# The normaliser multiplied into the gate on GpSimd: one multiplication moved off VectorE in a fused mLSTM and two-MLP kernel

## The reference, cut to what matters

```python
for t in range(S):
    m_new = np.maximum(f_gate[:, :, t] + m, i_gate[:, :, t])
    f_stab = np.exp(f_gate[:, :, t] + m - m_new)
    i_stab = np.exp(i_gate[:, :, t] - m_new)
    m = m_new
    C = f_stab[:, :, None, None] * C + i_stab[:, :, None, None] * np.einsum('bhd,bhe->bhde', vt, kt)
    n = f_stab[:, :, None] * n + i_stab[:, :, None] * kt
    h_tilde = np.einsum('bhde,bhe->bhd', C, qt)
    nq = np.einsum('bhd,bhd->bh', n, qt)[:, :, None]
    denom = np.maximum(np.abs(nq), 1.0)
    o = 1.0 / (1.0 + np.exp(-o_gate[:, :, t]))
    y[:, :, t] = o * h_tilde / denom
...
x = moe(x):  h = x @ w_in; g = np.maximum(0.01 * h, h); g @ w_out
x = moe2(x): h = x @ w_in; g = h * np.cos(h);           g @ w_out
```

## Time and profile before

| | |
|---|---|
| median of 3 runs | 845.6 us (844.89 to 846.51) |
| the profiled execution | 844.61 us, of it 842.9 in the span |
| TensorE busy | 832.1 us (99%) |
| VectorE, ScalarE, GpSimd busy | 626.5, 477.6, 309.2 us |

### The profile page before, as it was taken

One profiled execution on the slowest core, in us unless ns is written; L12 is line 12 of the kernel. 1 busy time (PEld: TensorE's weight loads), 2 busy tenths in 40 slices (PEclk: granted clock), 3 DMA queues, 4 the chain that ended last, 5 costly groups with the idle time before them and its releaser, 6 DMA issues.

```text
span 842.9 us, 15370 instructions
## 1 busy us (share of the span) xinstructions
PE 832.1 (99%) x5610; PEld 818.8 (97%) x5610; DVE 626.5 (74%) x1186; ACT 477.6 (57%) x1048; POOL 309.2 (37%) x340
## 2 busy tenths in 40 slices
PE   8999999999999999999999999999999999999997
PEld 7899999999999999999999999999999999999997
DVE  7598776676776666766654488888888888888886
ACT  6354433443433434334436687777777777777776
POOL 6764632222222332322005653333333333333332
PEclk9899999999999999999999999999999999999999
DMA  8764622434424224235013330301020202020000
GB/s 262 245 195 133 190 91 93 137 116 139 150 95 137 92 91 137 91 98 199 1 51 119 116 110 1 118 1 71 1 72 1 71 1 71 1 71 2 14 12 24
DMA packets 38450, 76.23 MB, mean 90 GB/s; under 512 B 3434, under 2 KB 27498, under 8 KB 38378
## 3 DMA queue, kind: packets, MB, share of 16 engines
q1 hardware_dynamic: 38330, 75.23, 27.4%
q10 hardware_dynamic: 48, 0.05, 0.0%
HBM read 63.28 MB, written 11.99 MB: 89 GB/s over the span
## 4 chain that ended last, share of the span: by engine, by line
PE 94%; DVE 1%; DMA 1%; ACT 1%; issue 1%; POOL 1%; SPq 0%; POOLq 0%; ACTq 0%; DVEq 0%
PE h L584 32%; PE acc L596 13%; PE acc L598 13%; PE acc L597 13%; PE s L584 10%; PE x L561 5%; PE s L507 3%; PE x L568 2%; PE x L549 2%; PE s L535 1%; DMA e_dram<-r_f 1%; DMA eG_b<-e_dram 1%; PE acc L658 0%; DVE w_in L1124 0%; ACT g_hi L710 0%
## 5 line engine op out<-in xcount | busy, mean ns | idle before, releaser
L584 PE MATMUL h<-xT,w_in 128*128 128x384 f32 x1536 | 303.4, 339 | 0.0
L584 PEld LDWEIGHTS h<-xT,w_in 128*128 128x128 f32 x1536 | 267.3, 188 | 0.3 <-DVE xT L1034 0.2
L710 ACT ACTIVATE t_f<-h 128x384 f32<-128x384 f32 x192 | 94.2, 490 | 293.3 <-PE h L584 293.2
L596 PE MATMUL acc<-w_out,g_hi 128*128 128x320 f32 x768 | 243.8, 317 | 2.1 <-POOL g_lo L1362 1.7
L598 PE MATMUL acc<-w_out,g_lo 128*128 128x320 f32 x768 | 237.4, 309 | 0.0
L597 PE MATMUL acc<-w_out,g_hi 128*128 128x320 f32 x768 | 236.1, 307 | 0.0
L1362 POOL TENSOR_TENSOR g_lo<-g_f,g_hi 128x384 fp32r<-128x384 f32 x127 | 130.0, 1024 | 212.2 <-ACT g_hi L710 212.2
L596 PEld LDWEIGHTS acc<-w_out,g_hi 128*128 128x128 f32 x768 | 144.4, 188 | 5.1 <-POOL g_lo L1362 1.9
L597 PEld LDWEIGHTS acc<-w_out,g_hi 128*128 128x128 f32 x768 | 144.4, 188 | 0.0
L598 PEld LDWEIGHTS acc<-w_out,g_lo 128*128 128x128 f32 x768 | 144.1, 188 | 0.0
L1049 DVE TENSOR_TENSOR g_f<-h,t_f 128x384 f32<-128x384 f32 x128 | 71.0, 555 | 96.7 <-ACT t_f L710 94.1
(11 more groups left out here) (130 smaller groups left out, 864.5 us busy)
## 6 DMA issues: line engine op xcount, KB each, us to landing
qk_s<-qk SPq DMA_DIRECT2D x24, 512.0 KB, 3.8
kvo_s<-kvo SPq DMA_DIRECT2D x24, 484.0 KB, 5.6
D<-g_dram SPq DMA_DIRECT2D x21, 512.0 KB
x_dram<-stage SPq DMA_DIRECT2D x8, 960.0 KB, 7.7
xT<-x_dram SPq DMA_DIRECT2D x8, 960.0 KB, 5.0
qe<-q SPq DMA_DIRECT2D x24, 180.0 KB, 4.2
out<-x SPq DMA_DIRECT2D x24, 160.0 KB, 1.8
raw_in<-w1i SPq DMA_DIRECT2D x8, 384.0 KB, 3.6
```

The lines of the kernel that those rows point to most:

```text
L584: last = nc.tensor.matmul(bank[:, 0:BLOCK], w(a), x[:, k, :], start=(n == 0), stop=(n == 7))
L596: nc.tensor.matmul(acc[t][:, 0:DM], g_hi[:, s, r], w_out[:, 0, j, :], start=(j == 0), stop=False)
L710: copy = lambda o, i, **k: nc.scalar.activation(o, i, ACT.Copy, **k)
```

## The change

VectorE's outputs are cut in two. normaliser (the three small instructions, now with a semaphore nrm_done) stands where the unit's output bank is ready. GpSimd gets a new function, gated, which multiplies the gate o_s in place by nrm, broadcast over the 40 columns, and counts gated_done. outputs waits for gated_done and multiplies the PSUM values by that product; the multiplication in PSUM is gone. In the slots the order on VectorE becomes normaliser, state, outputs. On GpSimd gated(b, c) stands at the end of unit_weights(b, c), and thus ahead of everything that belongs to the next unit. In the straight lists before slot 0 the calls are placed by hand.

```diff
-            def outputs(b, c):
+            def normaliser(b, c):
...
                 tt(nrm[:, p, :], o[:, :, HD], nrm[:, p, :], ALU.max).then_inc(nrm_step, 1)
-                dve.wait_ge(nrm_step, u * 4 + 2)
-                nc.vector.reciprocal(nrm[:, p, :], nrm[:, p, :]).then_inc(nrm_step, 1)
-                dve.wait_ge(nrm_step, u * 4 + 3)
-                o = o[:, :, 0:HD]
-                tt(o, o, nrm[:, p, :].unsqueeze(2).to_broadcast([P, HEADS, HD]), ALU.mult).then_inc(nrm_step, 1)
-                dve.wait_ge(nrm_step, u * 4 + 4)
-                dve.wait_ge(sig_done, u + 1)
+                dve.wait_ge(nrm_step, u * 2 + 2)
+                nc.vector.reciprocal(nrm[:, p, :], nrm[:, p, :]).then_inc(nrm_done, 1)
+
+            def outputs(b, c):
+
+                u, p = unit(b, c), c % 2
+                o = output_bank(b, c)[:, 0:HEADS * VD].rearrange("p (h d) -> p h d", h=HEADS)[:, :, 0:HD]
+                dve.wait_ge(gated_done, u + 1)
                 gate = o_s[:, c % BUFS, :].rearrange("p (h d) -> p h d", h=HEADS)
...
                 if u := row.unit(i, OUTPUTS):
+                    normaliser(*u)
                     state(*u)
                     outputs(*u)
...
+            normaliser(0, 0)
+            first_probs(2, (0,))
             outputs(0, 0)
-            first_probs(2, (0,))
             sigmoid(0, 2)
             first_probs(2, (1,))
             state(0, 1)
+            normaliser(0, 1)
+            x_lo(0, 0, xT[:, 0])
             outputs(0, 1)
-            x_lo(0, 0, xT[:, 0])
+            normaliser(0, 2)
+            x_lo(0, 1, xT[:, 0])
             outputs(0, 2)
-            x_lo(0, 1, xT[:, 0])
             x_lo(0, 2, xT[:, 0])
...
+            def gated(b, c):
+
+                pool.wait_ge(nrm_done, unit(b, c) + 1)
+                pool.wait_ge(sig_done, unit(b, c) + 1)
+                o = o_s[:, c % BUFS, :].rearrange("p (h d) -> p h d", h=HEADS)
+                nc.gpsimd.tensor_tensor(o, o, nrm[:, c % 2, :].unsqueeze(2).to_broadcast([P, HEADS, HD]), ALU.mult).then_inc(gated_done, 1)
...
                 if c > 0:
                     own_state(b, c - 1)
+                gated(b, c)
...
             own_state(0, 0)
+            gated(0, 0)
             first_mask(2, (1,))
             own_state(0, 1)
             first_scaled(2)
             first_keys(2)
+            gated(0, 1)
             split_in_lo(0)
+            gated(0, 2)
             second_columns()
```

More of the change, by code:

```diff
@@ L181, in build @@
         hm_done = sem("hm_done")
+        nrm_done = sem("nrm_done")
+        gated_done = sem("gated_done")
         ph_done = sem("ph_done")
@@ L991, in outputs @@
                 ts(nrm[:, p, :], o[:, :, HD], -1.0, 1.0, ALU.mult, ALU.max).then_inc(nrm_step, 1)
-                dve.wait_ge(nrm_step, u * 4 + 1)
+                dve.wait_ge(nrm_step, u * 2 + 1)
                 tt(nrm[:, p, :], o[:, :, HD], nrm[:, p, :], ALU.max).then_inc(nrm_step, 1)
-                dve.wait_ge(nrm_step, u * 4 + 2)
-                nc.vector.reciprocal(nrm[:, p, :], nrm[:, p, :]).then_inc(nrm_step, 1)
-                dve.wait_ge(nrm_step, u * 4 + 3)
-                o = o[:, :, 0:HD]
-                tt(o, o, nrm[:, p, :].unsqueeze(2).to_broadcast([P, HEADS, HD]), ALU.mult).then_inc(nrm_step, 1)
-                dve.wait_ge(nrm_step, u * 4 + 4)
-                dve.wait_ge(sig_done, u + 1)
+                dve.wait_ge(nrm_step, u * 2 + 2)
[4 more added lines that the diff above has]
+                dve.wait_ge(gated_done, u + 1)
                 gate = o_s[:, c % BUFS, :].rearrange("p (h d) -> p h d", h=HEADS)
```

## The result

| | before | after |
|---|---|---|
| median of 4 runs each | 846.0 us (844.89 to 846.51) | 866.0 us (862.53 to 867.87) |
| the profiled execution, its span | 844.61, 842.9 us | 867.79, 866.1 us |
| TensorE, VectorE, GpSimd busy | 832.1, 626.5, 309.2 us | 841.2, 628.0, 332.3 us |
| mean granted TensorE clock | 0.995 | 0.986 |

The change makes the kernel 2.4% slower: the ratio is 1.0238 [1.0217, 1.026]. Forecast were 854.2 us and a range up to 859.5. The direction was right, and the size was wrong by a factor of more than two.

The account below looks back on a forecast made before the run. TensorE, busy 832.1 of 842.9 us, was taken as the bound. Terms 2.25 + 2.7 + 1.8 + 1.8, say 8.6 us, on 844.61 gave 853.2, as median 854.2 us; ends 852.2 to 859.5, stated range 849.5 to 859.5.

Parts of the forecast that it names:

- the four places named: Before slot 0 and in slots 8, 9 and 13 of block 0: TensorE waits, 2.25, 2.7, 1.8 and 1.8 us.
- start, before slot 0: First three units: outputs wait for GpSimd's gate products, so qe and TensorE's first product come later, +2.25 us (1.6 to 3.8).
- slot 8, wait for D: Block 0: (0,3)'s gate product delays a w_out split and (0,4)'s decay work, so probabilities D come late, +2.7 us (2.0 to 4.2).
- slots 9 and 13, w_out: Block 0: w_out splits stand behind the gate products of (0,4) and (0,5), TensorE waits 1.8 us more each (1.5 to 2.2).
- load of (1,0): SyncE's queue after w_out: the data comes later but is covered by three and a half slots, 0 (0 to 1.5 us).
- units from (1,0) on: After block 0: GpSimd has 2.2 us to spare and VectorE's tile work is wanted two slots on, so 0.
- clock behind the new waits: TensorE's half clock after the new waits in block 0: nothing in the sum, 3.4 us only as rival 2.
- rival 2: Slot 8 of block 0: the clock falls in the gap, 6.8 us at half clock, 3.4 us less work, 857.6 us; chance 0.15.
- the fourth term: Slot 13 of block 0: split_out_lo(5) stands behind the gate product of (0,5), TensorE waits 1.8 us more for w_out.
- Rival 3: 18 later units: VectorE and GpSimd collisions use up the spare time, TensorE waits 0.3 us in each, +5.4, 859.6 us; chance 0.10.

Follow-up runs that it names:

- e1: Changed kernel's gate product on GpSimd for only the first three units, all others as in the kernel before: 847.62 us, ratio 1.0026.
- e12: The changed kernel with 13 warm-up matmuls instead of 2 ahead of the turn of (0,0): 862.87 us, ratio 1.0211.
- e8: The kernel before with 8 warm-up matmuls instead of 2 in TensorE's pause before unit (0,2): 841.88 us, ratio 0.9951.
- e2: Changed kernel's gate product on GpSimd for only units (0,3) to (0,5), all others as in the kernel before: 855.82 us, ratio 1.0125.
- e3: Changed kernel's gate product on GpSimd for only the 18 units from (1,0) on, block 0 as in the kernel before: 849.26 us, ratio 1.0041.
- e5: The changed kernel with unused identity products on TensorE ahead of four of its waits: 861.7 us, ratio 1.018.
- e4: The changed kernel with the load of (1,0) ahead of the last piece of w_out in SyncE's queue: 861.49 us, ratio 1.0182.
- e11: The changed kernel with the gate product of (0,4) moved behind piece 3 of w_out and that of (0,5) behind piece 5: 858.92 us, ratio 1.0169.
- e7: e3 with x_lo ahead of g_lo in VectorE's slot from block 1 on: 844.48 us, ratio 0.9979.
- e10: The kernel of e6 with the x_lo order of e7 and the 8 warm-up matmuls of e8: 842.53 us, ratio 0.9966.
- e6: Changed kernel, but first three units as before, later gate products placed behind GpSimd's next work, VectorE's state update first: 848.65 us, ratio 1.0038.
- e9: Changed kernel's gate product on GpSimd for only the first six units, on VectorE from (1,0) on: 859.87 us, ratio 1.0166.

## Why the prediction was wrong

**What held.** GpSimd lost its lead, and what stood behind its new waits came late, at the four places named. The forecast was 8.6 us, the loss was 20.0. Its lower end stands there twice, as 852.2 and as 849.5; the result lies above the upper end, 859.5, either way.

| step of the prediction | forecast | measured |
|---|---|---|
| start, before slot 0 | 2.25 | 2.0 (e1), 2.37 (e12 against e8), 3.1 in the change's profile |
| slot 8, wait for D | 2.7 | 2.57, and 0.74 on xT behind it |
| slots 9 and 13, w_out | 1.8 each | 1.52 each |
| load of (1,0) | 0 (0 to 1.5) | 2.52 (1.06 in e2) |
| units from (1,0) on | 0 | 3.5 (e3) |
| clock behind the new waits | 0 (3.4 as rival 2) | 6.8 in the profile, 4.3 by e5 |

The four terms that make the forecast's 8.6 measure 7.8 (2.2 + 2.57 + 3.04), so they were slightly too dear. (2.2 is the mean of e1 and e12. The first product came at 38.50 in the change's profile and not at 37.6: 0.5 us were lost ahead of the first gate product, where GpSimd's scaled queries began at 17.52 instead of 17.00 behind a load, and the half clock lasted 10.24 us instead of 6.83.) The error is in three steps that stood at nothing.

**The load of (1,0)**: "covered by the three and a half slots up to its scores" fails. I looked for the moment at which the data of (1,0) is read for the scores, and not for how far SyncE's queue would move. SyncE waits for the split of piece 5, which the fourth term itself had moved behind (0,5)'s normaliser. So its queue moved by 18.7 us, the lead that GpSimd lost, while TensorE was only 10.4 us late at (0,5). The first one who reads the load is GpSimd's logarithms. e4 and e11 cut the chain at two different links, and the wait disappears both times.

**The later units**: "the tile work behind it is wanted two slots on" fails. It holds for the tile work, but not for x_lo, which shares the slot and is wanted at once in slot 15. The numbers for it were at hand: g_lo at 2.51 against 0.55. Rival 3 had the mechanism with the wrong places, 18 units by 0.3 us; it was three by 1.16 us, 3.5 and not 5.4. The section of the Trainium skill that the prediction named ("SBUF — State Buffer", "SBUF: two separate sides") agrees with g_lo at 2.27 us beside GpSimd's work. It says that the two exclude each other, not who is hurt: that is the order of VectorE's queue, as e7 shows. Of the 12 us that were to leave VectorE nothing was seen either: its busy time went from 626.5 to 628.0 us, as g_lo took 13.3 us more. In e10, with GpSimd's lead kept, it was 615.6 us. The 0.74 us on xT in slot 8 are of the same family: TensorE's carried part of (0,4) writes the bank that x_lo of (0,3) reads, and x_lo stands behind the late probabilities in VectorE's queue.

**The clock** was rival 2, with a chance of 0.15 and one stretch. It should have been in the sum. The earlier trace rows showed that a pause of 1.8 us was followed by half clock; the argument against it, that TensorE does dense products between the waits of slots 8 and 9, was not borne out. But a pause of that length is not needed at the start: in e1, e5 and e6 the clock was at 0.50 from 23.7, 21.9 and 22.8 us on, before TensorE came to it, behind waits of 0.3 to 0.7 us. In all six profiles with an unfilled wait of 2.6 us in slot 8 (the change, e2, e4, e9, e11, e12) TensorE was at 0.50 behind it, for 3.41 to 13.65 us; with the wait filled (e5) it was at 1.00.

**The rest.** The parts measured apart make 17.7 us (e9 and e3), and the change loses 20.0. The mean clocks of its four runs fit a longer half clock in two of them: 867.79 and 867.87 us at 0.986, 864.28 at 0.990 and 862.53 at 0.992. From 0.986 to 0.992 is 0.6% of 866 us, 5.2 us of work, and the times lie 5.3 apart. The two better ones, at 18.3 and 16.5 us above the kernel before, are near what the parts give. That is argued from four runs, not shown by an experiment. Open is what decides in an execution whether half clock follows the wait of (1,0) and how long it lasts: it did in the change's profile and not in e9's, behind nearly the same wait.

## What to carry to other kernels

Where an engine that runs ahead gets a wait on a late result, its whole queue comes closer by the lead it had, not by the microseconds that the bounding engine loses: follow each queue that it feeds, a DMA queue too, to its first reader. When two elementwise engines come to lie beside each other, look in the slot for the small instruction that is wanted at once, and put it first. Price a new wait of TensorE with the half clock that may follow it, and look at the pauses that are already there: six more filler products in one gained 3.6 us, where the moved multiplications, in their best placing, gained nothing (e10 against e8).

## What the runs showed of the chip

- The stretch at half clock before slot 0 had different lengths with the same instructions there: 6.83 us in the kernel before, 10.24 in e3, 13.65 in e6. TensorE was busy nearly all that time (13.45 of 13.60 us in e6). The spread of runs goes with it: e8, with the clock at 1.00 throughout, has 12 runs within 0.8 us, and the 29 runs of the kernel before beside it lie between 843.3 and 854.5 us.
- TensorE's two waits of 1.52 us in slots 9 and 13, with large products on either side, were followed by half clock in no profile. Those of 1.8 to 1.9 us at the start, among small products, were in all four that have them (the kernel before, e2, e3 and e7). In three others (e1, e5 and e6) the half clock was there before the pause, behind waits of 0.3 to 0.7 us; e8 had waits of 0.48 and 0.70 us in the same place and stayed at 1.00. What tells them apart is open.
- Behind a pause filled with products that nobody needs TensorE stood at 1.00 in the profiles of all four kernels that had one (e5, e8, e10, e12). In their runs that holds for e8, all twelve at a mean clock of 0.999 or 1.000, and for seven of e10's nine.
- g_lo, 0.55 us when undisturbed, took 2.27 us in the changed kernel at 164.43, while GpSimd went through four instructions one behind the other (163.88 to 166.88); GpSimd's own last one, Cm 80x82, took 0.64 us instead of 0.33.
